# Where the narrowing products of a token group's last tiles stand, and in what order the next group's operands are made

## The chip, the cores and the metric

The kernel runs on one core of a Trainium2 chip. The metric is the device time of one execution in microseconds. A core has TensorE (PE), VectorE (DVE), ScalarE (ACT), GpSimd (POOL) and SyncE (SP, which here issues the transfers). Each engine runs its own instructions in the order in which they are written; semaphores order the engines against each other.

## The reference, cut to what matters

```
x   = masked_attention(q, k, v, proj)         # (2, 8, 768, 64), laid out as 1536 tokens x 512
g   = 1 / (1 + exp(-(x @ w_gate)))            # w_gate, w_val: 512 x 1536
x   = (g * (x @ w_val)) @ w_out               # w_out: 1536 x 512
h   = x @ w_in                                # w_in: 512 x 2048
g   = where(h >= 1, h, where(h <= -1, 0, (h + 1)**2 / 4))
out = g @ w_out2                              # w_out2: 2048 x 512
```

All in fp32. The change touches only what follows the attention.

## The kernel before

**Sets and groups.** The two feed-forward layers are worked off in 40 "sets". A set multiplies 256 columns of a widening weight by one group of 768 tokens. It does so by seven products r = 0 to 6 (`product(n, r)`, L715) of sums of blocks, in the manner of Strassen, in place of eight. Each operand is split into a high part (fp32r) and the remainder (low part), and a product is six matmuls of 384 columns (L729 to L731). Sets 0 to 23 are the first layer: even ones "gate", odd ones "value", six pairs for each of two token groups. Sets 24 to 39 are the second layer ("hinge"), eight for each group. `FIRSTS = (0, 12, 24, 32)` are the sets with which a group of tokens starts. There are three such changes of group within the stretch: 11 to 12, 23 to 24, 31 to 32.

**What a product needs.** Products alternate between two PSUM banks, so product r waits until product r-2 has been emptied (`emptied`). ScalarE empties product 0 (`first_product`, L954), VectorE all others (`empty`, L1246, product 4 in two instructions, L1239 and L1246). Products 0 and 1 of a set also wait for the set's weights, and all products of a set in FIRSTS for the token operands `xop`.

**Weights.** For each set GpSimd makes four sums (L488 to L495), ScalarE rounds the high parts (`round_w`, L928, L929, L931), and GpSimd subtracts to make the low parts (`low_a`, L500 and L502, which product 0 waits for; `low_s`, L506, which product 1 waits for). The output weights go the same way (L936 on ScalarE, L513 on GpSimd).

**Token operands.** The seven operands of a group are four sums (`sum_x`, VectorE, L1204 to L1214), seven roundings (`round_x`, ScalarE, L920) and seven remainders (`rest_x`, VectorE, L1193). They overwrite `xop` of the group before, so the rounding of r waits until product r of the last set is done.

**Hidden tiles and the narrowing product.** From a gate and a value set, or from one hinge set, come two tiles of 128 hidden columns by 768 tokens. The value set's are gated by `gate_quarter` and `gate_tiles` (L1259, L1265, L1267); the hinge set's are shaped by `clamp` (L1274), `hinge_part` (ScalarE, L965, L966) and `add_hinge` (L1278). Then each tile is rounded (`round_tile`, ScalarE, L946) and its remainder taken (`rest_tile`, VectorE, L1250). TensorE multiplies it by the output weights in "units": four units of six matmuls to a tile in the first layer (`down1`, L759, L760), six units of three matmuls in the second (`down2`, L770 to L772). They add up in the six other banks through a whole group. When a group's last tile is in, `empty_y` copies the banks to SBUF (VectorE L1283, L1284 or L1288; ScalarE L972, L973 or L977), and the next group's first tile waits for that.

**The order.** Everything is written out by hand. `units(n, r)` (L786) says how many units TensorE does behind product r of set n; `gate_set`, `value_set` and `hinge_set` write the order on ScalarE (L979 on) and VectorE (L1290 on). `down()` takes the units in one fixed sequence, so `units` decides how far the tiles run behind the sets. Before the change each set of the first layer carries four units, the tiles being one pair behind.

Of the kernel before, what the change touches and what calls it, by code (L numbers as in the profile page):

```python
# [22 lines left out]
def build(nc, q, k, v, proj, w_gate, w_val, w_out, w_in, w_out2, out):  # L23
# [39 lines left out]
    with ctx:  # L63
# [574 lines left out]
        def _(pe):  # L638
# [227 lines left out]
        def _(act):  # L866
# [112 lines left out]
            def gate_set(n):  # L979
# [3 lines left out]
                round_tile(2 * pp - 2)  # L983
                if after:
                    round_x(g, 5)
                    round_x(g, 6)
                round_tile(2 * pp - 1)
# [3 lines left out]
            def value_set(n):  # L991
# [14 lines left out]
                if n == FIRSTS[1] + 1:  # L1006
                    empty_y(0)
                if ahead:
                    for r in (2, 3, 4):
                        round_x(g + 1, r)  # L1010

            def hinge_set(n):
# [4 lines left out]
                round_tile(t - 2)  # L1017
                if n in FIRSTS:
                    round_x(g, 5)
                    round_x(g, 6)  # L1020
                if t - 1 > TILES1:
                    hinge_part(t - 1)
# [3 lines left out]
                round_tile(t - 1)  # L1026
# [13 lines left out]
                if ahead:  # L1040
                    round_x(g + 1, 4)
                if n in (N1, FIRSTS[3]):
                    empty_y(g - 1)
# [62 lines left out]
        def _(dve):  # L1106
# [173 lines left out]
            def empty_y(g):  # L1280
# [5 lines left out]
                else:  # L1286
                    dve.wait_ge(tile_used, TILES1 + T2)
                    dve.tensor_copy(osb[:, HT:T, :], ps[:, HT:T, :]).then_inc(y_dve, 1)  # L1288

            def gate_set(n):  # L1290
                t, g = 2 * pair_of(n), group_of(n)
                empty(n, 1)
                rest_tile(t - 2)
                empty(n, 2)
                if n in FIRSTS:
                    rest_x(g, 5)
                    empty(n, 3)
                    rest_x(g, 6)
                    rest_tile(t - 1)
                else:  # L1300
                    rest_tile(t - 1)
                    empty(n, 3)
                for r in (4, 5, 6):
                    empty(n, r)

            def value_set(n):
                g = group_of(n) + 1
                ahead = n + 1 in FIRSTS
                empty(n, 1)
                if ahead:  # L1310
                    sum_x(g, 0)
                    sum_x(g, 1)
                empty(n, 2)
                gate_quarter(n)
                if ahead:
                    rest_x(g, 0)
                empty(n, 3)
# [135 lines left out]
```

## Time and profile before

| | us |
|---|---|
| median of 3 runs | 828.76 (826.84 to 830.24) |
| profiled execution, its own time | 831.71 |
| span of its trace | 829.6 |
| TensorE busy | 789.2 |
| VectorE busy | 562.0 |
| GpSimd busy | 538.6 |
| ScalarE busy | 458.3 |

The profiled execution lies 2.95 us above the median of the runs, and 2.1 us of its own time lie outside the span. Set 1 starts at 261.76 us of the span; the sets fill the rest. In the trace a matmul's duration overlaps that of the next one, so what a matmul costs is read from the distance between two starts. "Idle before" at a row is the time its engine stood still, with the instruction that ended it. Window rows give, for each stretch, the busy time of each engine and the mean granted clock of TensorE (PEclk, 1.00 is full speed).

### The profile page before, as it was taken

How to read it: one execution, taken by the hardware profiler on the slowest of the kernel's cores; microseconds unless marked ns; L12 is line 12 of the kernel's file. 1: busy time of each engine (PE TensorE's matmuls, PEld its weight loads, DVE VectorE, ACT ScalarE, POOL GpSimd, SP SyncE). 2: the span in 40 equal slices, each digit the busy share in tenths (PEclk: the TensorE clock that was granted, in tenths of full speed). 3: DMA queues.
4: the chain of work that ended last, by engine and by line, in shares of the span. 5: the costliest groups of instructions: out<-in, count | busy, mean ns of one | idle time of the engine just before them, and what ended most of it. 6: DMA issues, size and time to landing. Idle time of an engine off the chain costs nothing.

```text
span 829.6 us, 12187 instructions
## 1 busy us (share of the span) xinstructions
PE 789.2 (95%) x4403; PEld 725.6 (87%) x4403; DVE 562.0 (68%) x867; ACT 458.3 (55%) x733; POOL 538.6 (65%) x529
## 2 busy tenths in 40 slices
PE   7999999999998999998899999988999989899998
PEld 6999999999787899997799999977899967799996
DVE  6888888887787545556765544686566797565564
ACT  4888988898885442333433323434555554544533
POOL 4666776776987977776765667476567775356520
PEclk9999999999999999999899999998999999999999
DMA  6897567544100222121011112001221120201002
GB/s 153 197 171 151 139 120 160 127 87 118 36 1 25 77 77 77 52 77 51 26 41 37 51 51 77 26 1 51 64 90 52 51 101 26 102 25 35 17 1 76
DMA packets 61930, 60.08 MB, mean 72 GB/s; under 512 B 28384, under 2 KB 51632, under 8 KB 61872
## 3 DMA queue, kind: packets, MB, share of 16 engines
q1 hardware_dynamic: 61712, 59.32, 27.4%
q8 instruction: 35, 0.57, 0.3%
q14 instruction: 23, 0.19, 0.1%
q10 hardware_dynamic: 160, 0.00, 0.0%
HBM read 37.75 MB, written 3.15 MB: 49 GB/s over the span
## 4 chain that ended last, share of the span: by engine, by line
PE 70%; DVE 14%; ACT 8%; issue 6%; POOL 1%; DMA 0%; SPq 0%; DVEq 0%; ACTq 0%; POOLq 0%
PE ps L729 10%; PE ps L730 10%; PE ps L731 10%; PE ps L759 8%; PE ps L771 5%; PE ps L770 5%; PE ps L772 5%; PE ps L760 4%; PE ps L695 4%; ACT ph L884 3%; DVE xop L1193 3%; ACT probs L888 2%; DVE probs L1168 2%; PE ps L712 2%; PE ps L683 2%
## 5 line engine op out<-in xcount | busy, mean ns | idle before, releaser
L729 PE MATMUL ps<-xop,wset 128*128 128x384 f32 x560 | 195.3, 349 | 24.9 <-DVE u L1246 8.4
L730 PE MATMUL ps<-xop,wset 128*128 128x384 f32 x560 | 192.5, 344 | 0.0
L731 PE MATMUL ps<-xop,wset 128*128 128x384 f32 x560 | 191.5, 342 | 0.0
L500 POOL TENSOR_TENSOR wset<-stage,wset 128x512 fp32r<-128x512 f32 x39 | 59.3, 1520 | 144.8 <-ACT wset L929 144.8
L1246 DVE TENSOR_TENSOR u<-ps,u 128x384 f32<-128x384 f32 x144 | 79.6, 553 | 106.7 <-PE ps L731 106.5
L729 PEld LDWEIGHTS ps<-xop,wset 128*128 128x128 f32 x560 | 107.3, 192 | 44.0 <-issue 12.5
L730 PEld LDWEIGHTS ps<-xop,wset 128*128 128x128 f32 x560 | 107.7, 192 | 3.8
L1179 DVE TENSOR_TENSOR pl<-ps,ph 128x768 fp32r<-128x768 f32 x96 | 91.5, 955 | 27.6 <-ACT ph L884 26.6
L731 PEld LDWEIGHTS ps<-xop,wset 128*128 128x128 f32 x560 | 107.6, 192 | 0.0
L475 POOL TENSOR_SCALAR probs<-probs,small 128x768 f32<-128x768 f32 x96 | 86.5, 908 | 25.6 <-DVE small L1173 22.8
L888 ACT ACTIVATE probs<-probs,small 128x768 f32<-128x768 f32 x96 | 90.0, 937 | 11.2 <-DVE probs L1168 10.8
L506 POOL TENSOR_TENSOR wset<-wsum,wset 128x1024 fp32r<-128x1024 f32 x39 | 95.6, 2451 | 0.0
L1168 DVE TENSOR_SCALAR_CACHE_REDUCE probs<-ps 128x768 f32<-128x768 f32 x96 | 90.9, 949 | 5.2 <-PE ps L686 4.7
L1246 DVE TENSOR_TENSOR hid<-ps,u 128x384 f32<-128x384 f32 x84 | 46.6, 555 | 67.6 <-PE ps L731 66.3
L884 ACT CAST ph<-ps 128x768 fp32r<-128x768 f32 x96 | 76.7, 800 | 20.4 <-PE ps L695 18.9
L695 PE MATMUL ps<-ident,probs 128*128 128x128 f32 x576 | 78.9, 273 | 1.9 <-DVE probs L1168 1.7
L954 ACT COPY u<-ps 128x384 f32<-128x384 f32 x40 | 19.2, 479 | 107.2 <-PE ps L731 107.0
L770 PE MATMUL ps<-wo,hh 128*128 128x512 f32 x192 | 75.9, 395 | 1.8 <-DVE hl L1250 1.8
L771 PE MATMUL ps<-wo,hh 128*128 128x512 f32 x192 | 76.3, 397 | 0.0
L772 PE MATMUL ps<-wo,hl 128*128 128x512 f32 x192 | 76.1, 396 | 0.0
L759 PE MATMUL ps<-hh,wo 128*128 128x512 f32 x192 | 76.0, 397 | 0.0
L695 PEld LDWEIGHTS ps<-ident,probs 128*128 128x128 f32 x576 | 67.2, 140 | 8.7 <-issue 4.3
(136 smaller groups left out, 1718.1 us busy)
## 6 DMA issues: line engine op xcount, KB each, us to landing
stage<-in_moe_w_in_dram SPq DMA_DIRECT2D x16, 512.0 KB, 4.0
stage<-in_moe_w_out_dram SPq DMA_DIRECT2D x14, 512.0 KB, 3.6
stage<-in_moe_w_gate_dram SPq DMA_DIRECT2D x12, 512.0 KB, 4.0
stage<-in_moe_w_val_dram SPq DMA_DIRECT2D x12, 512.0 KB, 3.4
ops<-qh SPq DMA_DIRECT2D x15, 384.0 KB, 5.3
ops<-kh SPq DMA_DIRECT2D x28, 192.0 KB, 5.3
qn<-in_q_dram SPq DMA_DIRECT2D x16, 192.0 KB, 4.5
kn<-in_k_dram SPq DMA_DIRECT2D x16, 192.0 KB, 5.6
```

The costliest lines, as they stand in the source:

```text
L695: last = pe.transpose(dst[:, t * P:(t + 1) * P], probs[n % RING][:, t * P:(t + 1) * P], ident[:, :])
L729: pe.matmul(dst, high[:, c, :], high_x(r)[:, c, :], start=(c == 0), stop=False)
L730: pe.matmul(dst, high[:, c, :], low_x(r)[:, c, :], start=False, stop=False)
L731: last = pe.matmul(dst, low[:, c, :], high_x(r)[:, c, :], start=False, stop=(c == 1))
L759: pe.matmul(main, w[:, cols], h[:, t % 3, 0:512], start=(first and n == 0), stop=(last_tile and n == 2))
L770: pe.matmul(ps[:, r, :], hh[:, t % 3, rows], wh, start=first, stop=False)
L771: pe.matmul(ps[:, r, :], hh[:, t % 3, rows], wl, start=False, stop=False)
L772: last = pe.matmul(ps[:, r, :], hl[:, t % 3, rows], wh, start=False, stop=last_tile)
L884: act.copy(dst, turned_slot("T", n).rearrange("p (t n) -> p t n", t=T)).then_inc(pt_high, 1)
L888: act.activation(probs[g % RING][:, :], probs[g % RING][:, :], ACT.Exp, bias=lowest(g), scale=-1.0, accum_out=total(g)).then_inc(exp_done, 1)
L1168: dve.tensor_scalar(probs[g % RING].rearrange("p (s n) -> p s n", s=2), score_slot(g), NO_MATCH, None, ALU.min, ALU.min, accum_out=lowest( ...
L1246: dve.tensor_tensor(dst, bank(n, r), other, ALU.add).then_inc(e_dve, 1)
```

## The change

`units` takes other numbers. The set before a change of group does seven products with no or few units between them (set 31 has two units behind products 0 and 1), and then all units of the tiles not yet multiplied in one block: 12 units (three tiles) behind sets 11 and 23, 24 units (four tiles) behind set 31. The first set of a group has no units, set 13 neither; sets 25 and 33 have eight, now from product 2 on. In other value sets the four units stand behind products 0, 1, 2 and 4, where they stood behind 0 to 3. The number of units is the same in all.

On VectorE and ScalarE the work follows: the last pair's two tiles are made in the set before the change of group instead of the one behind it; the remainders of the next group's first operands come after that set's emptyings, between the tiles; the first two sums are made one set earlier (`sums_ahead`); and `empty_y` moves to the start of the group's first set. On VectorE its copies of the third group now also wait for `x_low`, as ScalarE's did.

```diff
             def units(n, r):
+                ends = n + 1 in FIRSTS
+                if n < 2 or n in FIRSTS or n == FIRSTS[1] + 1:
+                    return 0
                 if n < N1:
-                    return int(n > 1 and (r > 2 if n % 2 == 0 else r < 4))
-                if n == N1:
-                    return (0, 0, 0, 2, 3, 3, 0)[r]
+                    if ends:
+                        return 3 * KT if r == R - 1 else 0
+                    return int(r > 2 if n % 2 == 0 else r in (0, 1, 2, 4))
+                if ends:
+                    return 4 * T if r == R - 1 else 2 if r < 2 else 0
                 if n in (N1 + 1, FIRSTS[3] + 1):
-                    return (0, 0, 0, 0, 2, 3, 3)[r]
-                if n == FIRSTS[3]:
-                    return (2, 2, 1, 2, 3, 3, 3)[r]
+                    return (0, 0, 1, 1, 2, 2, 2)[r]
                 return (2, 2, 1, 1, 2, 2, 2)[r]
```

On ScalarE, at the end of `value_set`:

```diff
                 if ahead:
-                    for r in (2, 3, 4):
+                    t = 2 * pair_of(n)
+                    round_x(g + 1, 2)
+                    round_x(g + 1, 3)
+                    round_tile(t)
+                    round_tile(t + 1)
+                    for r in (4, 5, 6):
                         round_x(g + 1, r)
```

On VectorE:

```diff
+            def rests_behind(n):
+                g = group_of(n)
+                empty(n, 1)
+                rest_x(g, 5)
+                empty(n, 2)
+                rest_x(g, 6)
+                empty_y(g - 1)
...
             def gate_set(n):
                 t, g = 2 * pair_of(n), group_of(n)
+                if n in FIRSTS:
+                    rests_behind(n)
+                else:
+                    empty(n, 1)
+                    rest_tile(t - 2)
+                    empty(n, 2)
+                    rest_tile(t - 1)
+                for r in (3, 4, 5, 6):
+                    empty(n, r)
+                sums_ahead(n)
...
             def value_set(n):
+                gate_tiles(n)
+                if n + 1 in FIRSTS:
+                    rest_tile(t)
                     rest_x(g, 0)
-                empty(n, 3)
-                if n == FIRSTS[1] + 1:
-                    empty_y(0)
-                if ahead:
                     rest_x(g, 1)
-                empty(n, 4)
-                if ahead:
+                    rest_tile(t + 1)
                     rest_x(g, 2)
                     rest_x(g, 3)
-                empty(n, 5)
-                if ahead:
                     sum_x(g, 2)
-                empty(n, 6)
-                if ahead:
                     sum_x(g, 3)
-                gate_tiles(n)
-                if ahead:
                     rest_x(g, 4)
```

`hinge_set` changes in the same way on both engines; in set 31 VectorE does `rest_x(0)`, `rest_tile(t)`, `add_hinge(t + 1)`, `rest_x(1)`, `rest_tile(t + 1)`, and then the rest, and in set 32 ScalarE does `empty_y(2)` ahead of `round_w(33)`.

VectorE behind the last widening of set 11 and in set 12, before the change (`u`, `hid` and `tmp` are where products are emptied to, `xt` a sum of token blocks, `xop` a token operand's remainder, `hl` a tile's remainder):

```order
L1246 TENSOR_TENSOR tmp<-ps,u3 128x384
L1211 TENSOR_TENSOR xt<-x 128x768
L1246 TENSOR_TENSOR u2<-ps,u2 128x384
L1214 TENSOR_TENSOR xt<-x,xt 128x768
L1265 TENSOR_TENSOR hid<-hid,tmp 128x768
L1267 TENSOR_TENSOR hid<-hid,u2 128x384
L1193 TENSOR_TENSOR xop<-xt,xop 128x768
L1246 TENSOR_TENSOR u2<-ps,u1 128x384
L1250 TENSOR_TENSOR hl<-hid,hh 128x768
L1246 TENSOR_TENSOR hid<-ps,u1 128x384
L1193 TENSOR_TENSOR xop<-xt,xop 128x768
```

The same place now, from the gating of the tiles to the last operand remainder ahead of set 12:

```order
L1275 TENSOR_TENSOR hid<-hid,tmp 128x768
L1277 TENSOR_TENSOR hid<-hid,u2 128x384
L1260 TENSOR_TENSOR hl<-hid,hh 128x768
L1203 TENSOR_TENSOR xop<-x,xop 128x768
L1203 TENSOR_TENSOR xop<-xt,xop 128x768
L1260 TENSOR_TENSOR hl<-hid,hh 128x768
L1203 TENSOR_TENSOR xop<-x,xop 128x768
L1203 TENSOR_TENSOR xop<-xt,xop 128x768
L1221 TENSOR_TENSOR xt<-x 128x768
L1224 TENSOR_TENSOR xt<-x,xt 128x768
L1203 TENSOR_TENSOR xop<-xt,xop 128x768
```

The remainders of operands 0 to 3, which stood between set 11's emptyings, now stand behind all of them, and both remainders of tiles (`hl`) stand ahead of the new group's emptyings.

VectorE in set 12 behind that, now:

```order
L1256 TENSOR_TENSOR u2<-ps,u1 128x384
L1203 TENSOR_TENSOR xop<-xt,xop 128x768
L1256 TENSOR_TENSOR hid<-ps,u1 128x384
L1203 TENSOR_TENSOR xop<-x,xop 128x768
L1293 COPY x<-ps 128x2x512
L1294 COPY x<-ps 128x2x256
L1256 TENSOR_TENSOR u3<-ps,u2 128x384
L1249 TENSOR_TENSOR hid<-ps,u3 128x384
```

The two copies of `empty_y`, which stood in set 13 ahead of the emptying of product 4, now stand in set 12 ahead of the emptying of product 3.

## Rows read from the trace of the kernel before

**Rows 1.** Page part 1: busy us, share of the span, instructions

```profile
PE 789.2 (95%) x4403; PEld 725.6 (87%) x4403; DVE 562.0 (68%) x867; ACT 458.3 (55%) x733; POOL 538.6 (65%) x529
```

**Rows 2.** Who TensorE waited for, 377 to 722 us: total us, times, longest

```profile
PE ps L729 <- DVE u L1246: 7.5, 7, 2.1
PE ps L729 <- DVE tmp L1246: 7.3, 2, 3.9
PE ps L729 <- DVE hid L1246: 5.7, 5, 1.9
```

**Rows 3.** Stretches of three sets: from:to length, busy us (x), granted clock, DMA

```profile
377.37:424.02 46.65, 39.28 (x200) 35.77 (x199) 35.33 (x39) 18.39 (x28) 31.36 (x24) 0.93 0.12 38
530.31:583.41 53.10, 46.21 (x224) 41.41 (x223) 38.88 (x48) 24.57 (x36) 31.36 (x22) 0.90 0.11 36
661.38:721.53 60.15, 51.91 (x236) 44.57 (x234) 46.55 (x53) 30.67 (x42) 36.41 (x29) 0.94 0.22 79
```

**Rows 4.** Stretches of single sets (1, 2, 4, 5, 27)

```profile
261.76:269.52 7.76, 7.71 (x43) 7.25 (x43) 4.84 (x9) 4.16 (x8) 6.37 (x7) 1.00 0.00 0
269.52:283.09 13.57, 12.56 (x70) 11.31 (x69) 9.25 (x12) 5.14 (x8) 13.35 (x12) 1.00 0.27 87
295.08:306.66 11.58, 11.58 (x67) 11.05 (x67) 7.26 (x12) 4.87 (x8) 7.95 (x7) 1.00 0.28 92
306.66:318.65 11.99, 11.93 (x69) 11.08 (x67) 4.50 (x7) 3.87 (x7) 10.01 (x10) 1.00 0.13 42
599.02:614.60 15.58, 15.58 (x80) 14.12 (x79) 9.96 (x13) 7.96 (x12) 10.46 (x10) 1.00 0.22 68
```

**Rows 5.** Timeline of TensorE: start us, us, instruction, idle before

```profile
295.08 0.34 PE L729 MATMUL ps<-xop,wset 128*128 128x384 f32 x1
299.25 0.39 PE L759 MATMUL ps<-hh,wo 128*128 128x512 f32 x1
...
393.44 0.47 PE L729 MATMUL ps<-xop,wset 128*128 128x384 f32 x1 [3.93 <-DVE tmp L1246]
...
394.35 0.53 PE L729 MATMUL ps<-xop,wset 128*128 128x384 f32 x1
394.67 0.53 PE L730 MATMUL ps<-xop,wset 128*128 128x384 f32 x1
```

**Rows 6.** Timeline of VectorE at set 11, 12 and 24

```profile
388.05 2.84 DVE L1193 TENSOR_TENSOR xop<-x,xop 128x768 fp32r<-128x768 f32 x1
...
392.75 0.55 DVE L1246 TENSOR_TENSOR tmp<-ps,u 128x384 f32<-128x384 f32 x1
...
404.98 3.14 DVE L1250 TENSOR_TENSOR hl<-hid,hh 128x768 fp32r<-128x768 f32 x1
...
552.03 0.95 DVE L1193 TENSOR_TENSOR xop<-xt,xop 128x768 fp32r<-128x768 f32 x1
```

**Rows 7.** Timeline of GpSimd at set 11

```profile
387.70 2.38 POOL L506 TENSOR_TENSOR wset<-wsum,wset 128x1024 fp32r<-128x1024 f32 x1
390.04 3.92 POOL L513 TENSOR_TENSOR wo<-stage,wo 128x512 fp32r<-128x512 f32 x2
```

**Rows 8.** Lines by form, 255 to 829 us: shapes xcount, busy us, mean ns

```profile
L1193 DVE TENSOR_TENSOR xop<-xt,xop 128x768 fp32r<-128x768 f32 x13 | 20.5, 1577 | 0.0
```

**Rows 9.** Timeline of VectorE: the group results copied out

```profile
420.06 1.22 DVE L1283 COPY x<-ps 128x1024 f32<-128x1024 f32 x1 [0.50 <-PE ps L760]
421.20 0.68 DVE L1284 COPY x<-ps 128x512 f32<-128x512 f32 x1
...
704.57 1.76 DVE L1288 COPY x<-ps 128x1536 f32<-128x1536 f32 x1 [1.53 <-PE ps L772]
```

**Rows 10.** Timeline of GpSimd beside the first of these copies

```profile
420.05 0.73 POOL L491 TENSOR_TENSOR wsum<-wsum,stage 128x256 f32<-128x256 f32 x1
```

**Rows 11.** Timeline of ScalarE: first weight rounding of set 14

```profile
413.02 0.62 ACT L928 CAST wset<-stage 128x512 fp32r<-128x512 f32 x1
```

**Rows 12.** Timeline of GpSimd: last weight remainder of set 14

```profile
415.96 2.42 POOL L506 TENSOR_TENSOR wset<-wsum,wset 128x1024 fp32r<-128x1024 f32 x1
```

More of the change, by code:

```diff
@@ L1025, in hinge_set @@
                     round_x(g + 1, 1)
-                round_tile(t - 1)
+                if n not in FIRSTS:
+                    round_tile(t - 1)
                 if n + 1 < NSETS:
@@ L1040, in hinge_set @@
                 if ahead:
-                    round_x(g + 1, 4)
-                if n in (N1, FIRSTS[3]):
-                    empty_y(g - 1)
+                    round_tile(t)
+                    hinge_part(t + 1)
+                    round_tile(t + 1)
+                    for r in (4, 5, 6):
+                        round_x(g + 1, r)
             act.dma_start(projn[0:D, :], proj).then_inc(proj_in, 16)
@@ L1313, in value_set @@
+                sums_ahead(n)
+            def value_set(n):
+                t, g = 2 * pair_of(n), group_of(n) + 1
+                empty(n, 1)
                 empty(n, 2)
                 gate_quarter(n)
-                if ahead:
+                for r in (3, 4, 5, 6):
+                    empty(n, r)
+                gate_tiles(n)
+                if n + 1 in FIRSTS:
+                    rest_tile(t)
                     rest_x(g, 0)
-                empty(n, 3)
-                if n == FIRSTS[1] + 1:
-                    empty_y(0)
@@ L1338, in hinge_set @@
-                ahead = n + 1 in FIRSTS
-                empty(n, 1)
-                rest_tile(t - 2)
+                t, g = 2 * pair_of(n), group_of(n) + 1
                 if n in FIRSTS:
-                    rest_x(g, 5)
-                if t > TILES1:
-                    add_hinge(t - 1)
-                if ahead:
-                    sum_x(g + 1, 0)
-                    sum_x(g + 1, 1)
-                empty(n, 2)
-                empty(n, 3)
-                if n in FIRSTS:
-                    rest_x(g, 6)
@@ L1352, in hinge_set @@
-                rest_tile(t - 1)
-                if ahead:
-                    rest_x(g + 1, 0)
-                    rest_x(g + 1, 1)
+                    rests_behind(n)
+                    empty(n, 3)
+                else:
+                    empty(n, 1)
+                    rest_tile(t - 2)
+                    if t > TILES1:
+                        add_hinge(t - 1)
+                    empty(n, 2)
+                    empty(n, 3)
+                    rest_tile(t - 1)
                 empty(n, 4)
-                if ahead:
-                    rest_x(g + 1, 2)
-                    rest_x(g + 1, 3)
@@ L1360, in hinge_set @@
                 empty(n, 5)
                 clamp(t)
-                if ahead:
-                    sum_x(g + 1, 2)
                 empty(n, 6)
-                if n in (N1, FIRSTS[3]):
-                    empty_y(g - 1)
                 add_hinge(t)
                 clamp(t + 1)
-                if ahead:
-                    sum_x(g + 1, 3)
-                    rest_x(g + 1, 4)
+                sums_ahead(n)
+                if n + 1 in FIRSTS:
+                    rest_x(g, 0)
+                    rest_tile(t)
+                    add_hinge(t + 1)
+                    rest_x(g, 1)
+                    rest_tile(t + 1)
+                    rest_x(g, 2)
+                    rest_x(g, 3)
+                    sum_x(g, 2)
+                    sum_x(g, 3)
+                    rest_x(g, 4)
```

43 lines of the change are left out of this document (14 added, 29 removed).

## The prediction

> **What bounds the kernel now.** I read the page's engine shares first: TensorE is busy 789 of 829.6 us [rows 1], so time can come only from TensorE standing still or running slowly. Next I listed whom TensorE waits for: between 377 and 722 us 7.5 + 7.3 + 5.7 = 20.5 us go to VectorE's emptyings [rows 2]. Last I cut the trace into stretches from set start to set start. A gate set with four units takes 11.58 us and a hinge set with twelve takes 15.58 [rows 4]. Four products take 299.25 - 295.08 = 4.17 us [rows 5], one product 1.04, seven 7.30. So a unit of the first layer is (11.58 - 7.30) / 4 = 1.07 us, of the second (15.58 - 7.30) / 12 = 0.69.
>
> With these prices the three changes of group should take:
> - sets 11 to 13: 3 x 11.58 = 34.74; they take 46.65. Lost 11.9.
> - sets 23 to 25: 21 products 21.9, 12 first-layer units 12.84, 8 second-layer units 5.52, together 40.26; they take 53.10. Lost 12.8.
> - sets 31 to 33: 21.9 + 36 x 0.69 = 46.74; they take 60.15. Lost 13.4.
>
> Sum 38.1 us [rows 3]. Some 20 of it is the waits. Another part is the clock: the three stretches have a granted clock of 0.93, 0.90 and 0.94. Only the levels 1.2 and 2.4 GHz occur, so the time at half speed is 2 x (0.07 x 46.65 + 0.10 x 53.10 + 0.06 x 60.15) = 24.4 us. Behind the wait of 3.93 us matmuls of 384 columns start 0.32 us apart instead of 1.04 / 6 = 0.174 [rows 5], so a microsecond at half speed loses 0.46, 24.4 at most 11.
>
> One small loss lies elsewhere: a value set takes 11.99 us, a gate set 11.58 [rows 4]. Its products 4, 5 and 6 stand without units between them, and product 6 waits for product 4's two emptyings.
>
> **Value sets.** With a unit behind product 4 product 6 starts 1.07 us later; two emptyings of 0.55 then fit. In exchange products 3 and 4 are adjacent, which asks only that products 1 and 2 be emptied, one unit earlier. I take the whole 0.41 us for each of the sets 3, 5, 7, 9, 15, 17, 19 and 21: 3.3 us. Bounds 0 and 3.3.
>
> **What VectorE's operations cost at a change of group.** An operation with two SBUF inputs takes 0.95 us alone (0.87 from start to start). Beside GpSimd it takes 2.84 or 3.14 [rows 6]: the first began 0.35 us into a remainder of 2.38 us on GpSimd [rows 7] and ended 0.8 us behind it. So it waits for GpSimd's running instruction to end. The mean of one form is 1.58 [rows 8]. An emptying reads PSUM and takes 0.55 even beside GpSimd's output-weight remainders of 1.96 each [rows 6, 7]. I reckon 0.87 plus the rest of GpSimd's instruction (0.7 for a sum, up to 2.4 for L506).
>
> **Sets 11 to 14.** Time 0 is the start of set 11. It now has no units, like set 1, which took 7.76 [rows 4]: 0.46 lost. The block needs its first tile at once (made in set 10), the second at 7.76 + 4 x 1.07 = 12.0. On VectorE: last emptying ends 8.4; first gating product 9.45 (behind L506); second 11.2 (behind one L513); the tile's remainder 13.35 (behind the other). TensorE waits 1.35. Then two operand remainders and the third tile's, each 0.87 + 0.7 behind GpSimd's sums: 18.0, needed at 17.6: 0.4. The block ends at 22.3, by which the operands 0 to 3 are made, and 4 at 23.1, which product 4 doesn't want before 26.5.
>
> Set 12 without units: VectorE does emptying 1 (from 2.3 us into the set, when product 1 is out), operand remainder 5, emptying 2, remainder 6, then the two copies, 1.22 + 0.68 [rows 9], then emptying 3, for which product 5 waits. 2.3 + 0.55 + 0.9 + 0.75 (product 2 is out) + 0.9 + 1.7 + 0.5 = 7.6 us, wanted at 5.2: 2.4 lost. Its cover is gone: the copies stood in a set with units. ScalarE's copies stand ahead of set 13's weights. From the first rounding of a set's weights to the last remainder 418.4 - 413.0 = 5.4 us pass [rows 11, 12], from about 4.1 us into set 12: 9.5, just when product 1 of set 13 would want it (9.75 + 1.04). Nothing is added. Set 13 is again a bare value set, 0.46. Set 14 follows as set 2 followed the bare set 1; set 2 took 13.57 [rows 4], 2 more than a gate set, with one weight set late. I take half: 1.0, less 0.4 that set 14 loses already.
>
> Sum: 0.46 + 1.35 + 0.4 + 2.4 + 0.46 + 0.6 = 5.7.
>
> **Sets 23 to 25.** The same, but GpSimd has no output weights there, so tile 22 is ready at 12.1 (0.15 late) and tile 23 in time: 0.46 + 0.15 + 2.2 for the copies in set 24. In set 25 first the hinge parts of set 24 stand ahead of `first_product` on ScalarE (0.85), then the first unit, now behind product 2 and not product 4, waits for tile 24 (1.45). Sum 5.1.
>
> **Sets 31 to 33.** In set 31 emptying 2 stands behind a tile remainder and an `add_hinge`, while only the first two products carry units: products 4 and 6 wait 1.15 and 1.0, and 0.15 at the end. The block of 24 units, 16.6 us, covers both tiles of set 31 and the operands. In set 32 the copy of 1.76 us [rows 9] costs 2.2. ScalarE's own copy waits for the last operand remainder and holds up the weights of set 33, whose product 1 wants them 1.3 us before they are there; tile and weights together cost 2.25 in set 33. Sum 6.75.
>
> **Bounds of the unseen.** These 17.5 us of waits are laid out by hand; no row shows a block. Below: if GpSimd never holds VectorE up and only the copies stay, 3 x 3.2 = 9.6. Above: each of some 12 two-input operations per change at 2.84 instead of 1.58 us.
>
> **Clock.** Instead of waits of up to 3.93 us I expect waits under 2.5. I take one spell at half speed per change, as long as half of those of the first stretch (2 x 0.07 x 46.65 / 2 = 3.3 us), 1.5 us each: 4.5. Bounds 0 and today's 11.
>
> The copies read PSUM and write SBUF. The one at 420.06 took 1.22 us although GpSimd worked from 420.05 to 420.78 with two SBUF inputs [rows 9, 10]. The Trainium skill (SBUF — State Buffer, "Who interferes with whom") counts `copy` among the operations that can take the port pair shared with GpSimd and then block for a whole instruction. [...]
>
> **Sum.** Waits 17.5 + clock 4.5 = 22 us lost where 38.1 are now: 16.1 gained. With 3.3 of the value sets 19.4. The profiled execution took 831.71 (span 829.6), so 812.3 for it. The median of the runs is 2.95 lower; I carry the difference over: 828.76 - 19.4 = 809.4.
>
> **Rivals.**
> - Nearly all is hidden: waits 9.6, clock full. 38.1 - 9.6 + 3.3 = 31.8 gained, 797. For it: the blocks of 12.8 and 16.6 us are long against the 10 us of VectorE work in them. Against: the copies keep their place on VectorE's queue, and the queue's work isn't less.
> - VectorE becomes the bound. It is busy 35.3 + 38.9 + 46.6 = 120.8 us in the three stretches [rows 3], nearly the 121.7 that TensorE needs. If it stands still 10 us in each, since emptyings can't be done ahead, they take 150.8 instead of 159.9: 9.1 + 3.3 = 12.4 gained, 816.4. The same comes out if the waits are as reckoned but hold the clock down as long as now (11 us lost instead of 4.5: 815.9). Beside this, the Trainium skill (TensorE: Matmul & The Clock Gate, "A second HAM failure mode: psum-queue depth-cycling") reports a clock that swings through short waits between matmul groups; by rows 3 to 5 long ones are the clearer cause here.
> - Slower: VectorE's dense queue meets GpSimd on each operation. Between set 11's last emptying and the copies 12 operations with two SBUF inputs follow each other, and the tiles' and product 3's are waited for. At a mean of 2.5 instead of 1.58 us this adds 11 us per change, 33 in all, 842. It decides from 0.65 us more per operation on, 2.2 us mean. Against: GpSimd's supply of work ends within the block (it waits for ScalarE's rounding of the next weights), and 1.58 is a mean over just these stretches.
> - No change: the block's saving and the bare sets' waits balance, 829.
>
> **Chances.** Forecast 0.60 (own range 803 to 815), all hidden 0.17, VectorE the bound 0.17, slower 0.03, no change 0.03. About 0.5%, 4 us, is what a measurement of this kernel can tell from no change. Faster by more: 0.60 + 0.17 + 0.16 = 0.93; within: 0.04; slower: 0.03. The range takes in most of the second and third case: 800 to 819.
>
> **What would show it.** Value sets of 11.6 us; the set before a change bare at 7.8 us with a block behind it; one wait of about 1.4 us at the second tile of the first block and almost none in the second; product 5 of the sets 12, 24 and 32 waiting about 2 us for the emptying behind the copies; set 33 waiting for weights; TensorE's total waits down from over 20 to some 17 us or less, and a granted clock of 0.95 or more in the stretches. It would be wrong if the blocks wait for several microseconds at each tile, if product 0 of the new group waits for operands, or if GpSimd's weights end last in sets 13 and 14.

## The result and the profile after

The changed kernel takes 820.94 us (median of 17 runs, 817.94 to 826.73), the kernel before in the same runs 829.55. The ratio is 0.9904, 95% interval 0.9886 to 0.9922: 8.0 us less by the ratio, 8.6 by the medians, where 19.4 were forecast. The direction was right; the time lies 2 us above the range of 800 to 819 us, 6 above the forecast's own of 803 to 815, and the gain is less than half of the forecast.

The page of the profiled execution (span 820.8 us): engine shares, the clock in 40 slices, and the shares of the chain that ended last. Before, TensorE was busy 789.2 us [rows 1].

```profile
PE 783.7 (95%) x4403; PEld 720.2 (88%) x4403; DVE 562.6 (69%) x867; ACT 460.0 (56%) x733; POOL 538.3 (66%) x529
...
PEclk9999999999999999999999999999999998999999
...
PE 61%; POOL 11%; DVE 9%; ACT 7%; issue 6%; DMA 5%; SPq 1%; DVEq 0%; POOLq 0%; ACTq 0%
```

A 9 stands for 90% or more, so the clock is read better from the stretches below: 1.00 and 0.96 in the first two, as forecast, and 0.92 in the third, where 0.95 or more was forecast. In the chain stand 11% GpSimd and 5% DMA, where before 1% and 0% stood. The forecast had neither.

Whom TensorE waits for from set 11 to 33 (total us, times, longest), against [rows 2]:

```profile
PE ps L729 <- DVE u L1256: 8.4, 4, 2.9
PE ps L770 <- DVE hl L1260: 7.1, 5, 3.1
PE ps L729 <- DVE hid L1256: 1.2, 2, 0.9
PE ps L759 <- DVE hl L1260: 1.1, 1, 1.1
PE ps L729 <- POOL wset L502: 0.9, 1, 0.9
```

A row of the kernel before, in the same stretch as [rows 2]:

```profile
PE ps L770 <- DVE hl L1250: 1.8, 1, 1.8
```

Waits of the products for VectorE fell from 20.5 to 9.6 us. Ahead of units of the second layer (L770) they grew from 1.8 to 7.1 us, 3.1 of them in one place, and there are new ones ahead of a unit of the first layer (L759) and for GpSimd's weights (L502). In all TensorE's waits fell from 22.3 to 19.0 us (0.3 of them for ScalarE); the prediction's sign was 17 or less.

The stretches of sets 11 to 13, 23 to 25, the sets 29 and 30, and the stretch of sets 31 to 33 (length, busy us, granted clock):

```profile
376.54:415.59 39.05, 36.04 (x201) 32.58 (x199) 31.36 (x39) 18.32 (x28) 27.76 (x22) 1.00 0.11 35
520.88:568.11 47.23, 43.02 (x224) 38.85 (x223) 38.12 (x46) 23.41 (x35) 27.95 (x21) 0.96 0.09 27
614.91:632.45 17.54, 16.11 (x79) 13.94 (x78) 10.58 (x13) 8.14 (x12) 11.02 (x10) 1.00 0.20 61
632.45:649.00 16.55, 15.98 (x79) 14.18 (x79) 10.48 (x13) 9.08 (x14) 11.32 (x10) 1.00 0.20 63
649.00:712.71 63.71, 53.58 (x236) 45.37 (x234) 45.60 (x51) 31.38 (x42) 36.12 (x29) 0.92 0.21 71
```

With the prediction's prices (34.74, 40.26 and 46.74 us for the three stretches) and against [rows 3]:

| | lost before | forecast | lost after |
|---|---|---|---|
| sets 11 to 13 | 11.9 | 6.6 | 4.3 |
| sets 23 to 25 | 12.8 | 6.6 | 7.0 |
| sets 29 and 30, above 15.6 each | 0 | 0 | 2.9 |
| sets 31 to 33 | 13.4 | 8.3 | 17.0 |

(Forecast: waits plus 1.5 us of clock; the 0.6 of set 14 are left out in the first line; set 14 took 12.36 us after 12.02.) The first two lines are about as laid out or better. The third change of group became worse than it was, and two ordinary sets ahead of it became slow. Together these two lines lie 11.6 us above the forecast; the first lies 2.3 below it, the second 0.4 above. Value and gate sets, below, brought 0.9 less than forecast, set 14 0.3 more. That is 10.3 of the 10.6 us by which this execution misses: 8.8 us of span gained instead of 19.4.

One execution is not the kernel, and two lines of this table are not steady. The sets 11 to 13 hold the same instructions in the profiles of five more runs below (swap_after, blocks_first_two, hinge_first, output_weights_first and tiles_first): they took 40.3 to 42.9 us there, so 39.05 is the best of six, and the loss is 4.3 to 8.2 us. The sets 29 and 30 hold the same instructions in hinge_first, output_weights_first and tiles_first, with the transfers in the old order, and lost 0, 0 and 1.5 us there. The third change of group lost 17 us or more in these three too, with their edits in set 31 (17.3, 20.2 and 18.4): that line is the one to explain.

A value set, against 11.99 in [rows 4]:

```profile
306.54:318.18 11.64, 11.64 (x68) 11.11 (x67) 4.50 (x7) 3.88 (x7) 9.79 (x10) 1.00 0.12 33
```

### The profile page after: what moved, and what is told of

Same layout as the page of the kernel before. It is cut to its first block, busy times and chain, and to the rows that moved or that the text cites. A ratio compares the mean times of both kernels' runs of the same rounds, so it can differ in the third digit from the quotient of the medians.

```text
span 820.8 us, 12188 instructions
## 1 busy us (share of the span) xinstructions
PE 783.7 (95%) x4403; PEld 720.2 (88%) x4403; DVE 562.6 (69%) x867; ACT 460.0 (56%) x733; POOL 538.3 (66%) x529
## 4 chain that ended last, share of the span: by engine, by line
PE 61%; POOL 11%; DVE 9%; ACT 7%; issue 6%; DMA 5%; SPq 1%; DVEq 0%; POOLq 0%; ACTq 0%
PE ps L729 9%; PE ps L730 9%; PE ps L731 9%; PE ps L759 8%; DMA stage<-in_moe_w_in_dram 4%; PE ps L760 4%; PE ps L695 4%; PE ps L770 3%; PE ps L771 3%; PE ps L772 3%; ACT ph L888 3%; ACT probs L892 2%; POOL wset L506 2%; DVE probs L1178 2%; PE ps L712 2%
## 5 line engine op out<-in xcount | busy, mean ns | idle before, releaser
L729 PE MATMUL ps<-xop,wset 128*128 128x384 f32 x560 | 192.7, 344 | 14.8 <-DVE u L1256 9.3
L730 PE MATMUL ps<-xop,wset 128*128 128x384 f32 x560 | 190.4, 340 | 0.0
L731 PE MATMUL ps<-xop,wset 128*128 128x384 f32 x560 | 190.0, 339 | 0.0
L500 POOL TENSOR_TENSOR wset<-stage,wset 128x512 fp32r<-128x512 f32 x39 | 59.6, 1527 | 133.3 <-ACT wset L933 133.3
L729 PEld LDWEIGHTS ps<-xop,wset 128*128 128x128 f32 x560 | 106.0, 189 | 30.3 <-issue 8.9
L730 PEld LDWEIGHTS ps<-xop,wset 128*128 128x128 f32 x560 | 106.4, 190 | 3.4
L731 PEld LDWEIGHTS ps<-xop,wset 128*128 128x128 f32 x560 | 106.0, 189 | 0.0
L506 POOL TENSOR_TENSOR wset<-wsum,wset 128x1024 fp32r<-128x1024 f32 x39 | 93.5, 2398 | 0.0
L888 ACT CAST ph<-ps 128x768 fp32r<-128x768 f32 x96 | 76.7, 801 | 20.5 <-PE ps L695 19.0
L770 PE MATMUL ps<-wo,hh 128*128 128x512 f32 x192 | 76.6, 399 | 7.1 <-DVE hl L1260 7.1
L759 PE MATMUL ps<-hh,wo 128*128 128x512 f32 x192 | 75.4, 397 | 1.1 <-DVE hl L1260 1.1
```

Source lines behind the costliest of these rows:

```text
L506: pool.tensor_tensor(weights(n, 1)[:, 3:7], wsum[:, :], weights(n, 0)[:, 3:7].bitcast(F32), ALU.subtract).then_inc(w_split, 1)
L729: pe.matmul(dst, high[:, c, :], high_x(r)[:, c, :], start=(c == 0), stop=False)
L730: pe.matmul(dst, high[:, c, :], low_x(r)[:, c, :], start=False, stop=False)
L731: last = pe.matmul(dst, low[:, c, :], high_x(r)[:, c, :], start=False, stop=(c == 1))
L759: pe.matmul(main, w[:, cols], h[:, t % 3, 0:512], start=(first and n == 0), stop=(last_tile and n == 2))
L770: pe.matmul(ps[:, r, :], hh[:, t % 3, rows], wh, start=first, stop=False)
```

## Where the time went: a ring through the transfer queue

GpSimd's waits in the second layer, sets 26 to 33, first of the kernel before, then of the changed one:

```profile
POOL wsum L488 <- DMA stage<-in_moe_w_in_dram: 30.6, 6, 5.2
```

```profile
POOL wsum L488 <- DMA stage<-in_moe_w_in_dram: 33.6, 6, 6.4
```

In each kernel GpSimd stands still six times for 5 us or more until a set's widening weights have landed. The row of the kernel before was there to be read and the prediction did not read it. The reason is in the order of SyncE: it issues the output weights `load_wo(n - N1)` after waiting for GpSimd's previous output-weight remainder, and the widening weights of the next set stand behind that in the same queue, although their buffer is free as soon as the weights of the set before last are split, about a turn earlier. So there is a ring: GpSimd's L513, two transfers, 4.5 to 6 us from its issue until the second lands, sums, ScalarE's roundings, L500 to L506, the next L513. One turn of it on GpSimd in the changed kernel, the longest:

```profile
617.14 2.02 POOL L513 TENSOR_TENSOR wo<-stage,wo 128x512 fp32r<-128x512 f32 x1
...
627.19 0.74 POOL L488 TENSOR_TENSOR wsum<-stage 128x256 f32<-128x256 f32 x1 [6.44 <-DMA stage<-in_moe_w_in_dram]
...
630.42 1.29 POOL L500 TENSOR_TENSOR wset<-stage,wset 128x512 fp32r<-128x512 f32 x1
...
634.72 2.02 POOL L513 TENSOR_TENSOR wo<-stage,wo 128x512 fp32r<-128x512 f32 x1
```

From the end of L513 at 620.7 us to the sums at 627.2 GpSimd stands still; from L513 to L513 the turn takes 634.72 - 617.14 = 17.6 us, more than TensorE's 15.6 for a set, because this transfer was waited for that long and the two L513 took 3.6 us together, where they took 2.9 at the same place before. SyncE's issues of widening weights at set 29, before and after:

```profile
632.04 0.47 SPq L385 DMA_DIRECT2D stage<-in_moe_w_in_dram  x1
```

```profile
621.18 0.47 SPq L385 DMA_DIRECT2D stage<-in_moe_w_in_dram  x1
```

Before, the next two issues follow 15.8 us after each other. It didn't matter there: the issue stands 632.04 - 630.20 = 1.8 us behind the start of set 29. That TensorE's long waits at the sets 24 and 25 had let the ring run ahead is the likely reason, not a tested one. In the changed kernel, where those two sets are shorter, the issue stands 621.18 - 614.91 = 6.3 us behind. In this execution TensorE had caught up with the ring and went at its pace. In hinge_first's profile it stands 4.0 us behind, and the sets 29 and 30 took 15.6 us.

What the ring did in set 31, in order: GpSimd's first sum for set 32, ScalarE's rounding of these sums, VectorE's `add_hinge`, TensorE's third tile of the block:

```profile
659.93 1.12 POOL L488 TENSOR_TENSOR wsum<-stage 128x256 f32<-128x256 f32 x1 [5.35 <-DMA stage<-in_moe_w_in_dram]
...
663.49 1.05 ACT L935 CAST wset<-wsum 128x1024 fp32r<-128x1024 f32 x1 [2.67 <-POOL wsum L495]
...
668.75 1.09 DVE L1288 TENSOR_TENSOR hid<-hid,tmp 128x768 f32<-128x768 f32 x1 [5.26 <-ACT tmp L970]
...
674.26 0.79 PE L770 MATMUL ps<-wo,hh 128*128 128x512 f32 x1 [3.07 <-DVE hl L1260]
```

ScalarE waits 2.7 us for GpSimd's sums. The hinge part of the tile stands behind this rounding in its queue, so VectorE waits 5.3 us for it, and TensorE 3.1 us for the tile. The stretch has a granted clock of 0.92, so some of it also ran at 1.2 GHz.

The copies cost about what the prediction said, 1.8, 2.9 and 1.9 us for 2.4, 2.2 and 2.2 (product 5 of the sets 12, 24 and 32, and the copy ahead of the last):

```profile
405.62 0.41 PE L729 MATMUL ps<-xop,wset 128*128 128x384 f32 x1 [1.78 <-DVE u L1256]
...
550.03 0.41 PE L729 MATMUL ps<-xop,wset 128*128 128x384 f32 x1 [2.87 <-DVE u L1256]
...
692.99 0.41 PE L729 MATMUL ps<-xop,wset 128*128 128x384 f32 x1 [1.91 <-DVE u L1256]
...
690.62 1.76 DVE L1299 COPY x<-ps 128x1536 f32<-128x1536 f32 x1
```

## The experiments

Two theories were set against each other first. Theory Q: the ring. Rival L: VectorE and GpSimd hold each other up on the port they share, and the third block's own work is too late whatever the transfers do. The ratio is to the kernel before, on the same chip.

### swap_after

```diff
-                if N1 <= n < FIRSTS[3]:
-                    sp.wait_ge(wo_split, T1 // 2 + n - N1)
-                    load_wo(wo2_v, n - N1)
+                if N1 < n <= FIRSTS[3]:
+                    sp.wait_ge(wo_split, T1 // 2 + n - 1 - N1)
+                    load_wo(wo2_v, n - 1 - N1)
```

> The changed kernel, but SyncE issues the widening weights of set n+1 ahead of its wait for the output-weight buffer, so that they no longer queue behind GpSimd's last output-weight remainder of the set before. Theory Q (the second layer is held by a ring: GpSimd's last remainder, then SyncE's two transfers, then 4.5 to 5 us until the weights land, then GpSimd again, some 16.3 us per set against 15.6 us that TensorE needs): GpSimd no longer waits 5 us per set for the transfer, sets 29 and 30 fall from 17.5 and 16.6 us to 15.6, set 31 loses 3 to 5 us instead of 9.4; in all 8 to 10 us less than the changed kernel's 820.9, so 811 to 813, ratio to before 0.978 to 0.981. Rival L (GpSimd and VectorE hold each other up on the shared port, output-weight remainders 3.6 us a pair instead of 2.9, and the third block's hinge work is too late by itself): unchanged, 820 to 822, set 31 still near 36 us.

814.5 us, ratio 0.980 (0.977 to 0.983). A set of the second layer, the stretch of the sets 31 to 33, and GpSimd's waits in the same part of the program:

```profile
605.15:620.72 15.57, 15.57 (x79) 14.12 (x78) 9.81 (x14) 8.29 (x12) 11.73 (x10) 1.00 0.21 69
651.90:707.61 55.71, 50.56 (x236) 43.32 (x234) 44.80 (x51) 29.75 (x40) 32.74 (x27) 0.97 0.21 73
```

```profile
POOL wset L500 <- ACT wset L933: 41.6, 8, 14.0
```

GpSimd no longer waits for a transfer at all. All ordinary sets take 15.6 us, and the third stretch loses 55.71 - 46.74 = 9.0 us, near the 8.3 laid out. All of the gain in it is set 31: 28.50 us for 36.47, while the sets 32 and 33 take 10.7 and 16.5 as without the swap. VectorE's wait for the hinge part falls from 5.3 to 2.0 us, TensorE's for the third tile from 3.1 to 0.4. The order of two transfers gives 6.4 us back by the medians and 8.6 by the ratios, whose intervals lie apart; the time stayed 1.5 us above the 811 to 813 expected. VectorE's and GpSimd's work is the same, though the swap also moves when GpSimd works beside VectorE. The chain of waits that goes away is what speaks for Q and against L. Part comes back elsewhere: the sets 23 to 25 took 49.2 us, where they take 47.1 to 47.4 in the five profiles with the same order and the old transfers. No run shows why.

### swap_before

The same edit in the kernel before.

> The kernel before with the same swap of transfers on SyncE and nothing else. Theory Q: the ring runs at 15.8 us per set there too, but the long waits at sets 24 and 25 give it a lead of 2 to 3 us over TensorE, so TensorE waits for it nowhere before set 31; 0 to 2 us less than before, ratio 0.998 to 1.000. Rival L: 0.

826.85 us, ratio 0.9963 (0.9946 to 0.9979): 3.1 us less, more than the 0 to 2 expected.

```profile
377.34:424.00 46.66, 38.52 (x200) 35.30 (x199) 35.34 (x39) 18.50 (x28) 31.37 (x24) 0.93 0.12 39
530.33:580.36 50.03, 43.01 (x224) 38.87 (x223) 38.54 (x47) 24.60 (x36) 30.15 (x23) 0.97 0.14 46
658.33:716.18 57.85, 51.58 (x235) 44.60 (x234) 44.42 (x53) 29.42 (x40) 34.05 (x28) 0.94 0.21 73
```

The first stretch is untouched; the second takes 50.03 instead of 53.10, with a granted clock of 0.97 for 0.90, the third 57.85 instead of 60.15. So the swap helps the kernel before too, by about half of what it gives the changed kernel. These stretches don't show where. In block_third's profile, without the swap, the sets 23 to 25 took 50.3 us at 0.97 (set 25 16.5 us at full clock, here 16.2, before 19.3 at 0.82), and in value_units' the sets 31 to 33 took 57.6: the differences of both stretches are ones that executions show without the swap.

### blocks_first_two and block_third

The order of before at some changes of group, of the changed kernel at the others: `NEW = (12, 24)` and `NEW = (32,)`, value sets as changed.

```diff
+                old = any(n in (f - 1, f, f + 1) for f in FIRSTS[1:] if f not in NEW)
...
-                    hinge_set(n)
+                    (old_hinge_set if old else hinge_set)(n)
```

> The change only at the sets 11 to 13 and 23 to 25 (and in the value sets); the sets 30 to 33 in the order of before. Theory Q: the first two changes of group save 7.6 and 5.9 us as in the changed kernel, value sets 2.4; but TensorE again catches up with the ring, sets 29 and 30 lose about 3 us and the third change of group loses 2 to 4 us more than the 13.4 of before: 818 to 821. Rival L, in which the third block is at fault by itself: sets 29 and 30 slow as well, but the third change of group at its 13.4 us: 815 to 817.

820.26 us, ratio 0.9879 (0.9849 to 0.9909).

```profile
376.31:416.62 40.31, 36.16 (x201) 32.70 (x200) 32.48 (x39) 18.30 (x28) 27.75 (x22) 1.00 0.11 34
521.93:569.04 47.11, 42.91 (x225) 38.74 (x224) 37.71 (x46) 23.79 (x36) 28.38 (x21) 0.96 0.08 26
647.40:709.03 61.63, 51.88 (x236) 44.51 (x234) 46.30 (x53) 31.01 (x42) 39.05 (x30) 0.94 0.22 77
```

The first two blocks alone bring all that the change brings. The third stretch, in the old order, took 61.63 us, 1.5 more than before, where Q expected 2 to 4; sets 29 and 30 lost only 0.4, where it expected 3. The time lay in Q's range, its two parts did not.

> The change only at the sets 30 to 33 (and in the value sets), the first two changes of group in the order of before. Theory Q: the ring has its lead of 2 us as before, sets 29 and 30 take 15.6 us, and the third change loses about the 8.3 us that the prediction laid out instead of 13.4: with 2.8 to 3.3 us of the value sets 820 to 823. Rival L: the third change loses 17 us as in the changed kernel, 829 to 831.

828.65 us, ratio 0.9977 (0.9957 to 0.9998), just below L's 829 to 831 and far from Q's 820 to 823. Set 31, and the wait for the block's third tile:

```profile
656.49:689.56 33.07, 29.11 (x127) 24.11 (x126) 25.54 (x27) 17.25 (x23) 19.54 (x15) 0.95 0.20 64
```

```profile
679.55 0.50 PE L771 MATMUL ps<-wo,hh 128*128 128x512 f32 x1 [3.09 <-DVE hl L1338]
```

The sets 29 and 30 took 15.6 us, as Q said, but the block still waited 3.1 us, and the third stretch lost 13.5 us: neither Q's 8.3 nor L's 17, but what it lost before the change. With the 4 us of the value sets in the time (value_units below) nothing is left for the third block. So the lead of the ring was not enough, and Q's statement that TensorE's catching up did the harm was too narrow. The chain ahead of the wait is the same as in the changed kernel: GpSimd waits 5.3 us for the weights of set 32, ScalarE 2.7 for its sums, VectorE 5.3 for the hinge part. The block uses set 31's tiles, and the last output weights, a set earlier than the order of before did, and the ring delivers for that order.

### value_units

The kernel before with

```diff
-                    return int(n > 1 and (r > 2 if n % 2 == 0 else r < 4))
+                    return int(r > 2 if n % 2 == 0 else r in (0, 1, 2, 4))
```

except in the value sets 1 and 13. The sets 11 and 23 have the new places too and took as long as before (16.1 and 15.5 us).

> The kernel before with one part of the change alone: in the value sets 3 to 9 and 15 to 21 the units stand behind products 0, 1, 2 and 4. By the term of the prediction, a value set falls from 11.99 to 11.6 us and eight of them give 2.8 to 3.3 us: 826 to 827, ratio 0.996 to 0.997. Rival: gate sets behind them lose it again (11.69 instead of 11.58 us in four of the changed kernel's), ratio 0.998 or more.

826.02 us, ratio 0.9954 (0.9932 to 0.9975), 3.8 us; a value set:

```profile
306.62:318.26 11.64, 11.64 (x69) 11.11 (x68) 4.50 (x7) 3.87 (x7) 9.80 (x10) 1.00 0.13 40
```

This term of the sum was about right. The eight sets give 8 x 0.35 = 2.8 us; four gate sets lose 0.1 each. The measured 3.8 us, with an interval of 2.1 to 5.6, is consistent with that.

### hinge_first

```diff
+                if ahead:
+                    hinge_part(t)
                 if n + 1 < NSETS:
                     round_w(n + 1)
...
-                hinge_part(t)
+                else:
+                    hinge_part(t)
```

> The changed kernel with its transfers as they are, but in set 31 ScalarE does the hinge part of the first tile ahead of the rounding of set 32's weights. Theory Q says that the late weights reach TensorE in set 31 only through ScalarE's queue: VectorE's wait of 5.3 us for the hinge part goes, the wait of 3.1 us ahead of the third tile of the block goes with it and perhaps a spell at half speed, while sets 29 and 30 stay at 17.5 and 16.6 us. Set 31 falls from 36.5 to 31 to 33 us, the whole to 816 to 818. Rival L (VectorE and GpSimd on the shared port make that tile late): set 31 stays above 35 us, 820 to 822.

822.49 us, ratio 0.9901 (0.9879 to 0.9924): no gain. VectorE's wait of 5.3 us for the hinge part fell to 1.2, as expected, but set 31 took 36.8 us. The sets 29 and 30, which were to stay at 17.5 and 16.6 us, took 15.6 each, though nothing up to them differs from the changed kernel. The wait ahead of the third tile in set 31 is now ended by another:

```profile
673.66 0.77 PE L770 MATMUL ps<-wo,hh 128*128 128x512 f32 x1 [3.79 <-POOL wo L513]
```

It waits for GpSimd's L513, the last output weights. They are the ring's last link, delayed further here since the weights' rounding was put back.

### output_weights_first

On top of hinge_first, on ScalarE and on GpSimd:

```diff
                     hinge_part(t)
+                    act.wait_ge(x_low, 3 * R)
+                    round_wo(T1 // 2 + n - N1, (narrow2(2 * (n - N1)), narrow2(2 * (n - N1) + 1)))
                 if n + 1 < NSETS:
                     round_w(n + 1)
...
+                if n == FIRSTS[3]:
+                    f = n - 1 - N1
+                    low_wo(T1 // 2 + f, f, (narrow2(2 * f), narrow2(2 * f + 1)))
                 sums_a(n)
```

> The changed kernel with its transfers as they are. In set 31 ScalarE does the hinge part of the first tile, then the rounding of the last output weights, then that of set 32's widening weights; GpSimd does the last output-weight remainder (L513) ahead of its four sums for set 32. Theory Q2 (formed after hinge_first: the ring's last link is the last pair of output weights, and the block of set 31 needs it one set earlier than the kernel before did, so the third tile of the block waits for it as well as for the hinge part): the wait ahead of that tile, 3.1 us in the changed kernel and 3.8 in hinge_first, falls under 1 us, set 31 from 36.5 to 31 to 33.5 us, the whole to 816 to 818. Rival L (VectorE on the shared port makes the tile late): the wait stays at 2.5 us or more, 820 to 822.

828.86 us, ratio 0.9976 (0.9951 to 1.0002): 6 to 8 us worse. GpSimd's remainder, ScalarE's rounding of set 32's sums, and the remainder of the third tile:

```profile
665.33 1.71 POOL L513 TENSOR_TENSOR wo<-stage,wo 128x512 fp32r<-128x512 f32 x1 [10.98 <-ACT wo L943]
...
671.92 1.04 ACT L938 CAST wset<-wsum 128x1024 fp32r<-128x1024 f32 x1 [5.84 <-POOL wsum L495]
...
675.20 1.73 DVE L1268 TENSOR_TENSOR hl<-hid,hh 128x768 fp32r<-128x768 f32 x1 [7.34 <-ACT hh L953]
```

The output weights were ready at 669.0, in time. But the sums of set 32 now stood behind them, ScalarE waited 5.8 us for those, and the tile's own rounding stood behind that: VectorE waited 7.3 us for it, TensorE 6.1 us for the third tile, and set 31 took 38.2 us. The edit moved the queue, so it didn't test the theory.

### tiles_first

Besides that:

```diff
                     round_wo(T1 // 2 + n - N1, (narrow2(2 * (n - N1)), narrow2(2 * (n - N1) + 1)))
+                    round_tile(t)
+                    hinge_part(t + 1)
+                    round_tile(t + 1)
                 if n + 1 < NSETS:
                     round_w(n + 1)
```

> The changed kernel with its transfers as they are, the last output weights ahead as in output_weights_first, and on ScalarE in set 31 also the rounding of both last tiles and the hinge part of the second ahead of every rounding of set 32's weights. In output_weights_first GpSimd's remainder of the output weights was done at 669.0 us, before TensorE wanted the third tile at 670.9, but the tile's own rounding stood on ScalarE behind a weight rounding that waited 5.8 us for GpSimd's sums; so that run moved the queue instead of removing it. Theory Q2 (the third block waits for set 32's late weights, through ScalarE's queue and through the output weights, not for VectorE's own work): with nothing of set 32's weights ahead of either, the wait before the third tile falls under 1 us and set 31 takes 31 to 34 us; the whole 815 to 819 us, ratio to before 0.983 to 0.988. If VectorE's own work and the shared port make the tile late (rival L), the wait is 2.5 us or more, 820 to 823.

822.45 us, ratio 0.9891 (0.986 to 0.9922). Set 31 and set 32, and what set 32 waited for:

```profile
649.57:682.48 32.91, 30.11 (x127) 25.74 (x127) 25.57 (x24) 16.25 (x22) 19.99 (x12) 0.90 0.15 48
682.48:695.86 13.38, 9.43 (x44) 8.66 (x43) 12.04 (x14) 5.98 (x8) 7.80 (x8) 0.87 0.13 41
```

```profile
677.57 1.05 ACT L938 CAST wset<-wsum 128x1024 fp32r<-128x1024 f32 x1 [1.76 <-POOL wsum L495]
...
688.40 0.41 PE L732 MATMUL ps<-xop,wset 128*128 128x384 f32 x1 [3.67 <-ACT u L961]
```

Set 31 came to 32.9 us and the third tile waited no more, as Q2 had it; the whole was not faster, where Q2 expected 815 to 819. ScalarE's rounding of set 32's sums, which waited until 677.57, now held up the token operands behind it, and TensorE waited 3.7 us for `first_product` in set 32. Three orders of the same work on ScalarE and GpSimd gave 822 to 829 us; only the earlier transfer gave 814.5.

### copies_last

From swap_after, VectorE's `empty_y` behind emptying 6 of the sets 12, 24 and 32.

```diff
                 rest_x(g, 6)
-                empty_y(g - 1)
...
                 for r in (3, 4, 5, 6):
                     empty(n, r)
+                if n in FIRSTS:
+                    empty_y(g - 1)
...
                 empty(n, 6)
+                if n in FIRSTS:
+                    empty_y(g - 2)
                 add_hinge(t)
```

> The kernel with the swapped transfers (814.5 us), and VectorE's copies of a finished group's result moved behind the last emptying of the sets 12, 24 and 32. The prediction's term says that they cost 1.9 to 2.9 us of waiting at product 5 of each. In set 12 all of it should go (set 12 from 10 to 12 us to 8), in sets 24 and 32 it goes too but the copies then stand ahead of the next tile, whose first unit stands behind product 2 of set 25 and 33, so 1 to 2 us come back there. In all 3 to 5 us less: 809.5 to 811.5. If the waits at product 5 come from the operand remainders and not from the copies: 814 to 815.

809.5 us, ratio 0.9755 (0.9732 to 0.9778): 5 us less than swap_after by the medians, 3.7 by the ratios, whose intervals overlap a little. The sets 12, 24 and 32:

```profile
397.82:405.78 7.96, 7.91 (x44) 7.17 (x43) 5.67 (x9) 5.41 (x9) 3.81 (x3) 1.00 0.00 0
540.85:549.86 9.01, 7.88 (x45) 7.20 (x44) 6.22 (x9) 4.99 (x9) 4.97 (x3) 1.00 0.01 2
672.25:682.04 9.79, 8.06 (x43) 7.00 (x41) 7.03 (x11) 4.72 (x7) 2.32 (x3) 1.00 0.00 1
```

They took 12.5, 10.8 and 10.7 us in swap_after's profile, the 12.5 partly at half speed (granted clock 0.80 over the set, 1.00 here); in the changed kernel's, at full clock, set 12 took 9.6. TensorE's waits of 2.9, 2.9 and 1.9 us for the emptying behind the copies are gone in the sets 12 and 32, and 1.1 us of waiting for an emptying is left in set 24. Part came back, as expected: set 25's first tile and set 33's first weights wait.

```profile
556.05 0.51 PE L770 MATMUL ps<-wo,hh 128*128 128x512 f32 x1 [2.15 <-DVE hl L1260]
...
682.04 0.44 PE L729 MATMUL ps<-xop,wset 128*128 128x384 f32 x1 [1.68 <-POOL wset L502]
```

### all_together

copies_last, with hinge_first's edit, the one of weights_before_copy, and:

```diff
-                    return (0, 0, 1, 1, 2, 2, 2)[r]
+                    return (0, 0, 0, 0, 2, 3, 3)[r]
```

> Swapped transfers, copies last, the hinge part first in set 31, in set 32 ScalarE's rounding of set 33's weights ahead of its own copy, and the units of sets 25 and 33 behind products 4 to 6 as before the change. Theory Q and the copies' term together: waits in set 33 fall by 1 to 2 us and in set 25 by 1 to 2 beside copies_last; 806 to 809, ratio 0.972 to 0.975. If the first tile's unit or the weights still come last in sets 25 and 33: 809 to 811.

816.07 us, ratio 0.9831 (0.9807 to 0.9856): worse than copies_last. Set 31 took 4.7 us more, with the same wait for L513 as in hinge_first (3.6 us), and set 25 took 18.1 us instead of 16.0. These are the places of hinge_first's edit and of the moved units, and together they are 6.8 us, where the medians differ by 6.6: what seemed a help was the harm.

### weights_before_copy

From copies_last, only ScalarE's copy in set 32 behind `round_w(33)`:

```diff
                     round_w(n + 1)
+                if n == FIRSTS[3]:
+                    empty_y(g - 1)
```

> copies_last (809.5 us), and in set 32 ScalarE rounds set 33's weights ahead of its own copy of the third group's result. In copies_last set 33 waits 1.7 us for GpSimd's L502 and 1.0 for L506. The prediction's term says that ScalarE's copy, itself waiting for the last operand remainder, holds these weights up: both waits go, 1 to 2.5 us less in the sets 32 and 33, the whole 807 to 808.5. If set 33's first tile then ends last instead: no difference, 809 to 810.

807.61 us, ratio 0.974 (0.9716 to 0.9763), the fastest version. Sets 32 and 33:

```profile
672.52:681.53 9.01, 7.92 (x43) 7.20 (x42) 6.22 (x9) 4.12 (x6) 6.23 (x4) 1.00 0.00 1
681.53:697.05 15.52, 13.65 (x68) 11.75 (x67) 11.86 (x16) 8.90 (x12) 9.12 (x10) 1.00 0.44 154
```

They took 9.79 and 16.08 in copies_last; both waits for GpSimd's weights are gone, and one of 1.5 us for set 33's first tile is there. The difference of the medians, 1.9 us, is in the forecast, but the intervals of the two ratios overlap.

## Why the prediction was wrong

**The step that failed** is the one on the sets 31 to 33: "The block of 24 units, 16.6 us, covers both tiles of set 31 and the operands." It went by VectorE's durations, with ScalarE and GpSimd free to start. In fact ScalarE's queue waits for set 32's weights, these for a transfer, the transfer for GpSimd's output weights of the set before. The prediction named SyncE's queue nowhere, and it read TensorE's waits only, not GpSimd's. Set 31 took 36.5 us, 9.9 more than its products and units cost (7.30 + 28 x 0.69 = 26.6); the prediction laid out 2.3 of waits. With the transfers swapped it took 28.5, 1.9 more. The whole stretch lost 17.0 us instead of 8.3, and 9.0 with the swap: so this omission is the cause at set 31, shown by swap_after. The sets 29 and 30 lost 2.9 us instead of 0 in this execution and nothing in two others of the same instructions, so they are no steady part of it. Set 33 waited 1.7 us for its first tile and not for its weights, where 2.25 were laid out for both. The medians put the gain of the swap at 6.4 us, not at the 10.9 us by which the two profiles differ in the sets 29 to 33: swap_after's took 3.9 us more in the sets 11 to 13, which the swap doesn't touch, and 2.0 more in the sets 23 to 25. Not run were the third block with the swap but without the first two blocks, and any other way to shorten the ring.

**Value sets**: 2.8 us, forecast 3.3, less 0.4 at the gate sets behind them, which the forecast didn't have. About right, and value_units alone gave 3.8 (2.1 to 5.6).

**Sets 11 to 14**: the bare set 11, the wait at the second tile (1.1 us, forecast 1.35), the wait of product 5 in set 12 (1.8 us, forecast 2.4 with a late product 2) and set 13 without added waits are as laid out. The third tile didn't wait. That the loss came out 2.3 us lower than forecast is in good part luck of this execution: in the six profiles with these instructions it is 4.3 to 8.2 us, with 6.6 forecast, and the wait of product 5 is 1.8 us in three and 2.9 in three.

**Sets 23 to 25**: 7.0 us, forecast 6.6. Product 5 waited 2.9 us (forecast 2.2), the first tile in set 25 1.25 (1.45).

**Copies**: the mechanism is right, and the size nearly (6.6 us of waits in all, 6.8 forecast). copies_last takes most of it away.

**Clock**: one spell per change was taken as 1.5 us. It is the least certain term: with the same instructions in the sets 11 to 13, the changed kernel's profile shows 39.05 us at 1.00, hinge_first's 40.5 at 0.96, and swap_after's 42.94 at 0.92:

```profile
376.30:419.24 42.94, 38.69 (x200) 35.37 (x199) 32.92 (x39) 18.39 (x28) 28.09 (x22) 0.92 0.10 31
```

**The rivals.** VectorE as the bound would have given 816.4, nearer to the result, but that would have been luck and not its mechanism: in swap_after and copies_last the same VectorE work fits into less time. The rival that needed GpSimd on each operation (842) didn't occur.

## What to carry to other kernels

When a stall that everybody waited through is removed, ask which queues had used it to run ahead, and measure their period against the new one: here a ring of 15.8 to 17.6 us stood hidden behind steps of 15.6 us while something else stopped them now and then. Read the waits of the engines that are not the bottleneck too, above all for transfers whose buffer is free; the cure is an order of issue, not a faster engine. And a block that pulls work forward by one step needs all its inputs forward by one step, output weights included; changing the order on ScalarE and GpSimd only passed the delay on in three runs.

## What the runs showed of the hardware

A transfer of the same 512 KB on the same queue took 4.6 to 4.9 us from issue to landing in four of the sets 26 to 31 of one execution and 5.7 and 5.9 us in two; nothing in these profiles says why. And whether a stretch with waits of 1 to 3 us has a spell at half speed differs between executions of the same code: 39.05 us for the sets 11 to 13 at a granted clock of 1.00 in one profile, 40.3 to 41.9 at 0.96 to 1.00 in four, 42.94 at 0.92 in another.
